# Moving the second weight split behind the hidden-tile work in the expert phase of an attention + MLP + routed-experts kernel

## The reference, cut to what matters

```
logits = x @ w_gate                    # x: (4352, 512)
e_idx = argmax(logits, axis=1)         # one expert per token
for e in range(8):
    mask = e_idx == e
    h  = maximum(x[mask] @ w1[e], 0)   # w1[e]: 512 x 1024
    ye = h @ w2[e]                     # w2[e]: 1024 x 512
    out[mask] = gate_w[mask] * eom[mask, e] * ye
```

## Time and profile before

| what | value |
|---|---|
| times of three runs | 1160.75, 1159.88, 1156.81 us |
| the profiled execution's own time | 1160.75 us |
| its span in the trace | 1158.9 us |
| TensorE busy | 1122.5 us (97% of the span) |
| VectorE, ScalarE, GpSimd busy | 648.0, 469.2, 77.0 us |
| mean granted TensorE clock | 0.986 |

### The profile page before, as it was taken

How to read it: one execution, slowest core, us unless ns; L and a number is a source line. 1 busy time by engine, 2 the same in 40 slices (tenths; PEclk the granted TensorE clock), 3 DMA queues, 4 the chain that set the end, 5 groups by cost and what they waited for, 6 DMA issues and landing times.

```text
span 1158.9 us, 20924 instructions
## 1 busy us (share of the span) xinstructions
PE 1122.5 (97%) x6358; PEld 888.2 (77%) x6359; DVE 648.0 (56%) x1247; ACT 469.2 (40%) x781; POOL 77.0 (7%) x96
## 2 busy tenths in 40 slices
PE   9999999999999999999999989799999999889996
PEld 7777777777777777777778978678888888767875
DVE  6575655655646556556564437466655445635642
ACT  4454444443444344434544342434443324424430
POOL 0000100101001001010010100010111101001111
PEclk9999999999999999999999989899999999998998
DMA  9210111112101110110020175688586445746551
GB/s 366 91 37 4 70 38 37 38 37 74 37 1 73 37 38 37 37 74 1 1 109 1 66 272 161 215 254 273 181 268 196 154 125 171 231 152 195 161 160 60
DMA packets 98784, 131.37 MB, mean 113 GB/s; under 512 B 13967, under 2 KB 75023, under 8 KB 94352
## 3 DMA queue, kind: packets, MB, share of 16 engines
q1 hardware_dynamic: 91360, 89.35, 24.4%
q10 hardware_dynamic: 1584, 23.07, 5.7%
q0 software_dynamic: 5760, 17.90, 4.0%
HBM read 85.86 MB, written 45.47 MB: 113 GB/s over the span
## 4 chain that ended last, share of the span: by engine, by line
PE 85%; DMA 4%; DVE 3%; SPq 2%; issue 2%; ACT 2%; ACTq 1%; POOL 0%; DVEq 0%; POOLq 0%
PE y_ps L855 33%; PE h_ps L837 15%; PE y_ps L928 14%; PE h_ps L912 6%; PE y_ps L912 6%; DMA hid_mv<-hidden 4%; PE a_ps L812 2%; PE h_ps L827 2%; SPq L609 1%; ACT we L1076 1%; PE a_ps L715 1%; ACTq L444 1%; PE a_ps L796 1%; SPq L574 1%; PE a_ps L776 1%
## 5 line engine op out<-in xcount | busy, mean ns | idle before, releaser
L855 PE MATMUL y_ps<-w_out_hi,hid_hi 128*128 128x512 f32 x544 | 217.5, 400 | 0.0
L855 PE MATMUL y_ps<-w_out_hi,hid_lo 128*128 128x512 f32 x544 | 212.2, 390 | 0.0
L855 PE MATMUL y_ps<-w_out_lo,hid_hi 128*128 128x512 f32 x544 | 212.0, 390 | 0.0
L928 PE MATMUL y_ps<-we,act_t_hi 128*128 (+1 forms) x608 | 190.3, 395 | 10.2 <-DVE act_t_lo L1560 5.2
L1365 DVE SCALAR_TENSOR_TENSOR hid<-hid,h_ps 128x512 f32<-128x512 f32 (+1 forms) x144 | 94.5, 656 | 166.2 <-ACT hid L1035 166.2
L837 PE MATMUL h_ps<-att_hi,mix 128*128 128x512 f32 x512 | 184.0, 402 | 0.1
L1035 ACT ACTIVATE hid<-h_ps,three 128x512 f32<-128x512 f32 (+1 forms) x144 | 95.6, 664 | 174.7 <-PE h_ps L837 151.3
L928 PEld LDWEIGHTS y_ps<-we,act_t_hi 128*128 128x128 f32 x608 | 115.8, 191 | 35.5 <-issue 11.4
L855 PEld LDWEIGHTS y_ps<-w_out_hi,hid_hi 128*128 128x128 f32 x544 | 102.1, 188 | 50.0 <-issue 30.4
L1374 DVE TENSOR_TENSOR hid_lo<-hid,hid_hi 128x512 fp32r<-128x512 f32 (+1 forms) x144 | 94.9, 659 | 70.6 <-ACT hid_hi L1043 70.1
L928 PE MATMUL y_ps<-we,act_t_lo 128*128 (+1 forms) x304 | 119.7, 394 | 0.0
(11 more groups left out here) (215 smaller groups left out, 1412.3 us busy)
## 6 DMA issues: line engine op xcount, KB each, us to landing
raw<-in_w ACTq DMA_DIRECT2D x11, 2048.0 KB, 9.2
hidden<-expert_hid SPq DMA_DIRECT2D x76, 256.0 KB, 3.1
hid_mv<-hidden SPq DMA_DIRECT2D x152, 128.0 KB
xg<-buckets SPq DMA_DIRECT2D x164, 64.0 KB, 2.0
xb<-in_x_rows SPq DMA_DIRECT2D x8, 1024.0 KB, 4.9
x_t<-in_x_t SPq DMA_DIRECT2D x7, 1024.0 KB, 4.8
buckets<-pad_row SPq DMA_DIRECT2D x8, 774.0 KB, 8.5
raw<-in_w SPq DMA_DIRECT2D x3, 2048.0 KB, 7.6
```

The lines of the kernel that those rows point to most:

```text
L855: i = pe.matmul(y_ps[:, t, :], (hid_hi, hid_lo)[hp][:, hid_at(b, j), t * P:(t + 1) * P], w_out_s[wp][:, j, :], start=(j == 0 and m == 0), ...
L928: i = pe.matmul(y2_ps[:, slot % 2, :], act_t[hp][:, slot % 2, f, :], we[:, bass.ds(w_at + (wp * WPART + KD * F + f * DM), DM)], start=(f = ...
```

## The change

On ScalarE, `hidden_hi(t-1)` is issued right after `rows_hi(t+2)`, ahead of the W2 split and of both places that load the next W2. On VectorE, `turn_hidden(t-1)`, `hidden_lo(t-1)` and `put_out(t-3)` come ahead of the W2 split. In VectorE's `body(0)` the three pieces of the first W2 come ahead of the first W1 split and of `turn_rows(2)` and `rows_lo(2)`. TensorE's, SyncE's and GpSimd's programs are as they were.

```
@@ scalar, body(t)
             if not t.first:
+                hidden_hi(t.plus(-1))
                 if is_b(t.n, 1):
                     load_w2(entry(act, Tile(0, MT), T_NEXT, E - 1), 1)
...
                     split_hi(1, n, other)
                     with act.If(split2 > 1):
                         load_w2(entry(act, before_it, T_NEXT, E - 1), n + 1)
-                hidden_hi(t.plus(-1))
@@ vector, body(t)
+            if t.first:
+                split_lo(dve, 1, 0, 0, range(1, PIECES), "w2_ready")
             with dve.If(split1 > 0):
                 split_lo(dve, 0, ..., signal="w1_ready")
             if not (isinstance(t.n, int) and t.n + 2 >= MT):
                 turn_rows(t.plus(2))
                 rows_lo(t.plus(2))
-            if t.first:
-                split_lo(dve, 1, 0, 0, range(1, PIECES), "w2_ready")
             if not t.first:
+                turn_hidden(t.plus(-1))
+                hidden_lo(t.plus(-1))
+                if not (isinstance(t.n, int) and t.n < LAG2):
+                    put_out(t.plus(-LAG2))
                 before_it = t.plus(-1)
                 with dve.If(split2 > 0):
                     split_lo(dve, 1, ..., signal="w2_ready")
-                turn_hidden(t.plus(-1))
-                hidden_lo(t.plus(-1))
-                if not (isinstance(t.n, int) and t.n < LAG2):
-                    put_out(t.plus(-LAG2))
```

More of the change, by code:

```diff
@@ L1579, in body @@
                              signal="w2_ready")
[L1580 to L1583, removed]
         def finish(t):
```

## The result

The change is slower. Its median is 1164.29 us (1163.56 to 1165.76, 8 runs) against 1158.35 us of the kernel before (1152.46 to 1160.98, 8 runs): a ratio of 1.006, 95% interval 1.0037 to 1.0083, some 6 to 7 us. The prediction was 1158.8 us and no clear change; the number is near that of its rival B (1166 us, a chance of 0.22), whose sign, a stall of `first(15)`, is absent. The profiled execution took 1164.95 us, its span is 1163.2 us.

A forecast was written before the change was run, and what follows sets the result against it. TensorE was taken as the bound, its few stalls and the slower clock behind them as what could change. Terms +1.0, +4.7, 0, +2.4, -9.2 and 0 gave -1.1 us: 1159.6 against the profiled 1160.75, median 1158.8, range 1151 to 1167.

The forecast's parts named there:

- rival B: Load's wait for w2_ready delays relu and next bounce, so each W2 split adds a stall: +6, 1166 us; chance 0.22.
- a stall of `first(15)`: Sign at tile 12's W2 split: if first(15) stalls too, the forecast is wrong and rival B holds.
- The front: Start of expert phase: first(2) stalls some 3.6 us plus 1.9 of clock; second(0) doesn't wait, TensorE 4.2 us ahead.
- Tile 3: Its W2 split: first(6) stalls over 4 us plus 1.9 of clock, losing the lead; +1.0 us together with the front.
- Tile 7: Its W2 split: first(10) can start only at 814.5 instead of 810.68; +4.7 us, bounds 0 and +7.
- Until here ScalarE and VectorE are where they were: At tile 7's W2 split: the hidden tile is read at T = 800.86, as in the kernel before.
- Tile 12: Its W2 split: T+13.6 meets TensorE's own delayed time, 870.8; 0 us, bounds 0 and +2.5.
- Tile 25: Its W2 split: the W1 split in body 27 comes later, first(28) waits 5.9 us instead of 3.5; +2.4 us.
- Tile 28: Its W2 split: second(27) stalls 0.8 us instead of 4.3, first(32) no longer stalls; -9.2 us.
- Tile 31: Its W2 split: no load behind it and no stall before or after; 0 us.
- The price of the clock: TensorE's granted clock falls behind long stalls: 1.9 us added behind each stall over 2 us.

The follow-up runs named there:

- g1: The kernel before with the change's order only in the loop's fourth body (W2 splits of tiles 7 and 31): 1163.28 us, ratio 1.0039.
- f2: The kernel before with ScalarE's weight loads cut to 128 of 4096 columns (times only, not a usable program): 1144.61 us, ratio 0.9881.
- f3: The change with ScalarE's weight loads cut to 128 of 4096 columns (times only, not a usable program): 1144.47 us, ratio 0.9872 to the kernel before.
- g4: The change, but with the old order in the loop's first body (tiles 12 and 28): 1171.99 us, ratio 1.0104 to the kernel before.
- g2: The kernel before with the change's order only in the loop's second body (W2 split of tile 25): 1162.92 us, ratio 1.0033.
- e2: The kernel before with only ScalarE's body(1) as in the change, hidden_hi(0) ahead of the second W2 load: 1155.44 us, ratio 0.9961.
- f1: The change with the next W2 load moved into the next body, behind relu and rows_hi: 1161.99 us, ratio 1.0014 to the kernel before.
- e3: The kernel before with the change's order at every W2 split, without its two front edits: 1171.54 us, ratio 1.0089.
- e4: The kernel before with the change's order only in the loop's first body of four (W2 splits of tiles 12 and 28): 1155.82 us, ratio 0.9962.
- e1: The kernel before with only VectorE's body(0) as in the change, three W2 pieces ahead of tile 2's rows: 1156.22 us, ratio 0.9983.
- f4: The kernel before with ScalarE's body(1) as in the change and the change's order at tiles 12 and 28: 1152.38 us, ratio 0.994.
- g3: The kernel before with ScalarE's body(1) as in the change; a table flag puts hidden work first only at a single-tile expert's W2 split: 1169.93 us, ratio 1.0083.

## Why the prediction was wrong

- *The front (VectorE's body(0), ScalarE's body(1)).* Right: `first(2)` stalls 3.4 us (3.6 was said) and runs partly at the lower clock, at a price of 2.9 us (1.9 was said); the bounce of tile 0 is read 5.2 us after its issue, at 723.6, and `second(0)` doesn't wait.
- *Tile 3.* Right in kind and inside its bounds: a stall of 4.4 us (over 4), +2.2 us in all (+1.0). `first(6)` starts 0.6 us later than forecast, and the clock behind the stall costs 2.5 us instead of 1.9.
- *Tile 7.* This is the step that failed, the term "+4.7 us". It measured +8.5 in the change, over its upper bound of +7. That the split behind the bounce stalls `first(10)` was right (g1, f2 and f3 show it). What was wrong is above all the start of the string, "Until here ScalarE and VectorE are where they were": the bounce was read 4.2 us later, counted from `first(0)` (98.2 against 93.9). Of this, 1.9 us is that the W1 load was issued later (86.26 against 84.31): by then the front and tile 3's split had made ScalarE about as late as TensorE. In g1, without them, the read is 0.4 us late and not 4.2. The other 2.3 us is that the load took 11.9 us from its issue to the read (791.0 to 802.9), where I took the 9.6 us of the earlier trace rows. g4, whose order is that of the change up to here, has 9.6 us again (793.30 to 802.90), so this part differs from run to run and isn't shown to be the change's. Smaller was the length, 14.5 us and not 13.6: behind the issue of the load ScalarE takes 2.5 us to the relu (812.37 to 814.86), where I took 1.9, and 1.5 us to the start of the split, where I took 0.9. The sum closes: `first(10)` ends 10.7 us late instead of 5.7, by 4.2 + 0.9 us and 0.1 less of clock, and 1.2 of these 5.0 us stand at tile 3 already.
- *Tile 12.* Right: 0.
- *Tile 25.* The direction was right; +4.1 instead of +2.4. The bounce was read 0.5 us later than TensorE's own lateness explains, the string to `turn_hidden(25)` was 13.8 us and not 13.2, and what is behind it 0.5 us longer. Alone (g2) it costs 3.8 us.
- *Tile 28.* Right in kind, -8.1 instead of -9.2: no stall at all before `second(27)`, but 1.6 us before `first(32)`. ScalarE's wait for `y2_ps` is 9.1 us and delays only the split.
- *Tile 31.* Right: -0.3.

The terms missed by +1.2, +3.8, 0, +1.7, +1.1 and -0.3 us, 7.5 in all (+6.4 instead of -1.1). The median is off by only 5.5 us (1164.29 against 1158.8), mostly because `first(0)` happened to start 2.2 us earlier in this profile, and that is luck. The base of the forecast, three executions with a median of 1159.88, was 1.5 us above the median of eight.

The price of the clock, "1.9 us behind each stall over 2 us", was no constant. In the change it was 2.9, 2.5, 1.8 and 1.6 us, and it didn't grow with the stall. It was nothing (5.7 us for the block, granted clock 1.00) behind a stall of 3.5 us before `first(4)` in e2, and 1.9 us behind one of 1.9 us before `second(6)` in f1 (granted clock 0.77).

Rival B named the load's wait for `w2_ready`. f1 shows the load with its wait to be about 2 us of each string. But B's condition, a string of 15 us and more and stalls at tile 12 too, didn't come: the strings are 14.0 to 14.5 us and `first(15)` doesn't stall. That its number is near is in good part luck.

## What to carry to other kernels

Work that is not urgent is best placed where the engine would wait in any case, and behind what is urgent where it wouldn't: ask of each place not which of two steps is more urgent, but what the engine would be waiting for in between. An order that is right where one dependency is late (the split of a single-tile expert) can be wrong everywhere else, so cut such a change by place before judging it. Where two engines and a queue wait for each other in a string, take the length of the string from a place where it is seen whole, and carry the lateness that one place makes over to the start of the next string, on every engine and not on one alone.

## What the runs showed of the hardware that was not expected

Whether the bounce of tile 0 lands in 5 or in 11 us is a matter of 0.2 us. SyncE's issue of its four transfers takes 2.67 us. Where the 2 MB load on ScalarE's queue was issued at most 0.05 us after the end of that, the tile is read 11.3 to 11.9 us after the first issue (the kernel before, e3, g1, g2). Where the load was issued 0.23 or 0.28 us after it, the tile is read after 5.5 and 5.1 us (e4, e1). Two profiles, with SyncE's issue of the bounce, ScalarE's issue of the load and VectorE's read; e3:

```profile
721.02 2.67 SPq L609 DMA_DIRECT2D hid_mv<-hidden  x4
```

```profile
723.54 0.39 ACTq L1126 DMA_DIRECT2D raw<-in_w  x1
```

```profile
732.39 1.31 DVE L1556 STREAM_TRANSPOSE act_raw<-hid_mv 128x512 f32<-128x512 f32 x2 [8.19 <-DMA hid_mv<-hidden]
```

and e4:

```profile
720.88 2.67 SPq L609 DMA_DIRECT2D hid_mv<-hidden  x4
```

```profile
723.78 0.39 ACTq L1126 DMA_DIRECT2D raw<-in_w  x1
```

```profile
726.35 1.30 DVE L1556 STREAM_TRANSPOSE act_raw<-hid_mv 128x512 f32<-128x512 f32 x2 [1.92 <-DMA hid_mv<-hidden]
```

That both cases occur in the kernel before would explain why its times spread over 8.5 us (1152.5 to 1161.0), while those of the change, where the load always comes later, keep within 2.2 us. The other runs go mostly with it: where the load is in its old place the times spread over 6.1 to 10.4 us (e1, e3, e4, g1, g2), where it comes later over 1.8 to 3.7 (e2, f1, g4), but 5.7 and 5.6 in f4 and g3. The one profile of the kernel before is of its slower end (1160.75 us), so this is argued and not shown.
